# Gated linear attention: exponents formed on TensorE in PSUM, output weights as the loaded operand, decay applied to token rows, scores on 64-row halves, gate rows in three parts

## The chip, the cores and the metric

The kernel is one program on 1 core of one Trainium2 chip. The metric is the time of one execution on the device in microseconds, the median of several. The core has TensorE (PE; matmuls from SBUF into PSUM, each with a weight load shown as PEld), VectorE (DVE), ScalarE (ACT), GpSimd (POOL) and SyncE (SP, which here only starts DMAs). Each engine runs its own list of instructions in order; they meet at semaphores.

## The reference, cut to what matters

```python
# attention: q, k, v, o_gate (2, 8, 768, 40), i_gate, f_gate (2, 8, 768)
for t in range(S):
    m_new = np.maximum(f_gate[:, :, t] + m, i_gate[:, :, t])
    f_stab = np.exp(f_gate[:, :, t] + m - m_new)
    i_stab = np.exp(i_gate[:, :, t] - m_new)
    m = m_new
    C = f_stab[..., None, None] * C + i_stab[..., None, None] * einsum('bhd,bhe->bhde', vt, kt)
    n = f_stab[..., None] * n + i_stab[..., None] * kt
    h_tilde = einsum('bhde,bhe->bhd', C, qt)
    denom = np.maximum(np.abs(einsum('bhd,bhd->bh', n, qt)), 1.0)
    y[:, :, t] = sigmoid(o_gate[:, :, t]) * h_tilde / denom
# x = y with the heads side by side: (2, 768, 320)
h = np.maximum(x.T @ w_tok1, 0) @ w_tok2        # over tokens
u = x + h.T
u = u + np.maximum(u @ w_ch1, 0) @ w_ch2        # over channels, 1536 wide
gate = sigmoid(causal 5-tap convolution of u with conv_w)
out = (gate * (u @ w_val)) @ w_out
```

## The kernel before

**Attention.** The recurrence is done in chunks of 128 tokens: `NC` = 6 for each of the 2 batches; chunk `u` = 6 b + n. The 8 heads stand in two groups `g` of four: group 0 on rows 0 to 39, group 1 on rows 64 to 103. The gate rows, 16 heads by 768 tokens, are scanned by VectorE in two parts (`ROWS_PARTS`): `m_row` the running maximum, `G_row` the summed log decay since the chunk's start, `A_row` the log weight of each token, `W_row` the weight up to the chunk's end. `G_row` goes to DRAM and comes back broadcast to 128 rows (`G_all`). For each chunk then:

- VectorE forms the exponents of the 128x128 matrix of each head, `min(G_all + A_col, mask)`, eight instructions (L933); ScalarE takes the exponential (L697).
- TensorE forms scores from zero-padded 128-row `k_in` and `q_in` (L1209, in `s_ps`), VectorE multiplies them with the exponentials (L952, `prob`).
- The chunk's output is `hv_ps`, stored as 41 values (40 and the normaliser) by 128 tokens: the 41 columns of `v_in` (L1194) and of the state `apart` (L1190, against `qs`, the queries times `decay`, GpSimd L590) are loaded, `prob` or `qs` is streamed, group 1 writes PSUM rows 64 and up. ScalarE copies it (`ht`, L712), TensorE turns it (`turn_y`, L1230), VectorE normalises it (L972 to L982), GpSimd multiplies by the output gate (L602), and it is split into a rounded part and a rest (`y_hi`, `y_lo`).
- The state gets `wv` by keys (L1220, job `delta`) plus `kept`, the old state times the chunk's decay.

**The rest.** Token mixing (`token_hidden` L1246, `token_skip`, `token_mixed`), the channel products in steps of 128 of 1536 hidden channels (`channel_hidden` L1171, job `ch1`; `channel_out` L1309), then convolution, `val` and `out`. Each product is three fp32r products of hi and lo parts. Weights arrive in ten pieces and are split by ScalarE (hi) and VectorE or GpSimd (lo, `make_lo`).

**Order.** Everything is written out by hand. The first batch's attention runs first, with token products of finished chunks between; the second batch's seven attention steps stand behind every second channel step of the first quarter `q` = 0 (`ATT_AT`). Two PSUM banks `shared` are handed round in the order of the list of `shared_bank_jobs`: job number N waits at `begin` until job N-2 has been released with `took`.

## Time and profile before

| | us |
|---|---|
| median of 3 runs | 311.26 (309.58 to 311.6) |
| span of the profiled execution, first to last instruction | 308.2 |
| TensorE busy | 270.8 |
| VectorE busy | 210.7 |
| ScalarE busy | 121.9 |
| GpSimd busy | 89.4 |

The profiled execution is known by its span alone; what the device time has around it is the difference to the median, 3.1 us. A busy matmul time counts each matmul from its start to its modelled end, so overlapping ones look long; how far apart starts lie is the better price.

### The profile page before, as it was taken

Reading aid. Unit: us, or ns where it says so; the run is one execution under the profiler, and the core shown is the slowest. Engines: PE = TensorE matmul, PEld = TensorE weight load, DVE = VectorE, ACT = ScalarE, POOL = GpSimd, SP = SyncE. Lnnn points to the kernel's source line nnn. Section 1 sums busy time; section 2 is a strip of 40 time slices with the busy share of each in tenths; the row PEclk is TensorE's granted clock in tenths of the full one; section 3 lists DMA queues with packets and bytes.
Section 4 is the critical chain, followed back from the end, with each engine's and each line's share of the span. In section 5 each row is a group of like instructions: output and inputs, shape, how many; then the busy total and the mean of one; then the engine's idle time right before and its main releaser. Section 6 shows DMA issues by size and latency. Waiting matters only on the chain.

```text
span 308.2 us, 5374 instructions
## 1 busy us (share of the span) xinstructions
PE 270.8 (88%) x2024; PEld 258.5 (84%) x2024; DVE 210.7 (68%) x415; ACT 121.9 (40%) x224; POOL 89.4 (29%) x102
## 2 busy tenths in 40 slices
PE   0876765884999999999999999999999999999854
PEld 0765654783998999999899999999999999999754
DVE  7999999977778687576677740352774138763693
ACT  4344453432874453434434223323123333231623
POOL 4537445554046445334610400000004000040340
PEclk9999598796899999999999999999999999999999
DMA  7599833344547554242000001000000010000011
GB/s 223 158 309 310 241 128 83 100 170 144 169 128 217 141 155 117 66 136 65 2 0 0 3 0 66 0 0 2 0 2 1 32 34 0 2 0 1 23 43 64
DMA packets 26289, 25.70 MB, mean 83 GB/s; under 512 B 13976, under 2 KB 22008, under 8 KB 26264
## 3 DMA queue, kind: packets, MB, share of 16 engines
q1 hardware_dynamic: 21976, 18.72, 20.9%
q10 hardware_dynamic: 4288, 6.64, 6.5%
q8 instruction: 16, 0.26, 0.3%
q14 instruction: 9, 0.07, 0.1%
HBM read 23.34 MB, written 2.02 MB: 82 GB/s over the span
## 4 chain that ended last, share of the span: by engine, by line
PE 60%; DVE 17%; issue 7%; ACT 6%; DMA 4%; POOL 3%; SPq 1%; ACTq 0%; DVEq 0%; POOLq 0%
PE shared L1171 25%; PE h_ps L1309 18%; DVE prob L933 7%; PE s_ps L1209 3%; DVE gate L1037 2%; PE hv_ps L1190 2%; PE shared L1274 2%; PE s_ps L1246 2%; PE hv_ps L1194 2%; PE shared L1230 2%; DVE y_lo L942 1%; DMA G_all<-G_scratch 1%; PE shared L1259 1%; DMA stage<-val 1%; DMA stage<-wout 1%
## 5 line engine op out<-in xcount | busy, mean ns | idle before, releaser
L933 DVE SCALAR_TENSOR_TENSOR prob<-G_all,A_col,mask_sb 128x128 f32<-128x128 f32 x96 | 51.3, 602 | 0.2 <-DMA G_all<-G_scratch 0.2
L1101 DVE SCALAR_TENSOR_TENSOR h_lo<-shared,h_hi 128x384 fp32r<-128x384 f32 x48 | 26.5, 557 | 35.0 <-ACT h_hi L826 34.8
L1309 PE MATMUL h_ps<-ch_hi,h_hi 128*128 128x320 f32 x144 | 45.4, 315 | 0.0
L1309 PE MATMUL h_ps<-ch_hi,h_lo 128*128 128x320 f32 x144 | 44.5, 309 | 0.0
L826 ACT ACTIVATE h_hi<-shared 128x384 fp32r<-128x384 f32 x48 | 23.1, 488 | 53.8 <-PE shared L1171 50.8
L1309 PE MATMUL h_ps<-ch_lo,h_hi 128*128 128x320 f32 x144 | 44.3, 308 | 0.0
L697 ACT ACTIVATE prob<-prob 128x512 f32<-128x512 f32 x24 | 15.0, 631 | 48.5 <-DVE prob L933 48.4
L1171 PE MATMUL shared<-u_hi,ch_hi 128*128 128x384 f32 x96 | 32.9, 342 | 0.6 <-DVE yt L982 0.4
L1171 PE MATMUL shared<-u_lo,ch_hi 128*128 128x384 f32 x96 | 32.5, 339 | 0.0
L1171 PE MATMUL shared<-u_hi,ch_lo 128*128 128x384 f32 x96 | 32.5, 338 | 0.0
L1037 DVE SCALAR_TENSOR_TENSOR gate<-x,conv_sb,gate 128x384 f32<-128x384 f32 x44 | 29.0, 668 | 1.0
L1209 PE MATMUL s_ps<-q_in,k_in 128*128 128x128 f32 x192 | 27.2, 301 | 2.1 <-DMA q_in<-qT 2.1
L1209 PEld LDWEIGHTS s_ps<-q_in,k_in 128*128 128x128 f32 x192 | 25.3, 212 | 4.1 <-DMA q_in<-qT 2.2
L1309 PEld LDWEIGHTS h_ps<-ch_hi,h_hi 128*128 128x128 f32 x144 | 27.1, 188 | 0.4 <-DVE yt L982 0.2
L1309 PEld LDWEIGHTS h_ps<-ch_lo,h_hi 128*128 128x128 f32 x144 | 27.1, 188 | 0.0
L1309 PEld LDWEIGHTS h_ps<-ch_hi,h_lo 128*128 128x128 f32 x144 | 27.0, 188 | 0.0
L1194 PE MATMUL hv_ps<-prob,v_in 128*41 128x128 f32 x192 | 20.6, 309 | 2.3 <-DVE prob L952 2.3
L952 DVE TENSOR_TENSOR prob<-s_ps,prob 128x512 f32<-128x512 f32 x24 | 15.8, 686 | 7.4 <-PE s_ps L1209 7.1
L602 POOL TENSOR_TENSOR y<-yt,o_sig 128x320 f32<-128x320 f32 x11 | 11.4, 1033 | 31.3 <-DVE yt L982 31.3
L1171 PEld LDWEIGHTS shared<-u_hi,ch_hi 128*128 128x128 f32 x96 | 18.0, 188 | 1.5 <-DVE yt L982 0.7
L536 POOL TENSOR_TENSOR ch_lo<-stage,ch_hi 128x640 fp32r<-128x640 f32 (+1 forms) x8 | 13.2, 1661 | 20.7 <-ACT ch_hi L668 20.7
L1230 PE MATMUL shared<-ident_r,ht 105*128 105x105 f32 x48 | 7.4, 282 | 12.5 <-ACT ht L712 12.5
(189 smaller groups left out, 620.6 us busy)
## 6 DMA issues: line engine op xcount, KB each, us to landing
G_all<-G_scratch SPq DMA_DIRECT2D x11, 512.0 KB, 4.8
o_sig<-on ACTq DMA_DIRECT2D x2, 960.0 KB, 6.1
k_in<-kT SPq DMA_DIRECT2D x24, 80.0 KB
q_in<-qT SPq DMA_DIRECT2D x24, 80.0 KB
kn_in<-kn SPq DMA_DIRECT2D x12, 160.0 KB, 3.9
v_in<-vn SPq DMA_DIRECT2D x12, 160.0 KB, 4.6
stage<-ch ACTq DMA_DIRECT2D x3, 640.0 KB, 4.4
out<-o_sb SPq DMA_DIRECT2D x12, 160.0 KB, 1.8
```

The source lines that it names most:

```text
L536: eng.tensor_tensor(lo[:, half], raw[:, half], hi[:, half].bitcast(F32), ALU.subtract).then_inc(split[p], 1)
L697: act.activation(prob[w % 4][:], prob[w % 4][:], ACT.Exp).then_inc(exp_ready, 1)
L826: act.activation(h_hi[i % 3][:], ps_of(key)[:, 0:T], ACT.Relu).then_inc(hi_ready, 1)
L933: last = dve.scalar_tensor_tensor(out=prob[(2 * u + g) % 4][:, tile_cols(j)], in0=G_all[u % 2][:, tile_cols(h)], scalar=A_col[:, col:col + ...
L952: dve.tensor_tensor(prob[w % 4][:], s_ps[g][:], prob[w % 4][:], ALU.mult).then_inc(prob_ready, 1)
L1037: return dve.scalar_tensor_tensor(out=gate[:, d, :], in0=xt, scalar=w, in1=gate[:, d, :], op0=ALU.mult, op1=ALU.add)
L1101: took(dve.scalar_tensor_tensor(out=h_lo[i % 3][:], in0=ps_of(key)[:, 0:T], scalar=0.0, in1=h_hi[i % 3][:].bitcast(F32), op0=ALU.max, op1= ...
L1171: last = pe.matmul(out_ap, w, x, start=(n == 0), stop=(n == len(terms) - 1))
L1194: last = pe.matmul(hv_ps[64 * g:64 * g + D1, tile_cols(j)], v_in[v % 3][:, g * HG + j, :], prob[(2 * v + g) % 4][:, tile_cols(j)], start=( ...
L1209: last = pe.matmul(s_ps[g][:, tile_cols(j)], k_in[k_buffer(u)][:, g, tile_cols(j)], q_in[k][:, tile_cols(j)], start=True, stop=True)
L1230: last = pe.transpose(ps[:, j * P:j * P + 64 + D1], ht[:, tile_cols(j)], ident_f[0:64 + D1, 0:64 + D1])
L1309: last = pe.matmul(h2_ps[t][:, 0:DM], a[:, tile_cols(t)], w[:, f, :], start=(f == 0 and n == 0), stop=(f == FT - 1 and n == 2))
```

## The change

What it does, by part:

- **Exponents.** G_all, the DRAM round trip, A_col and the eight VectorE instructions go. TensorE adds the mask (identity loaded, mask streamed) and the two gate terms (`AB`, 66 rows, loaded; `MV`, 66 rows by 1024, streamed: head indicators and two flat rows with the rounded G and its rest, filled by two DMAs from `GH`). ScalarE reads the exponents from PSUM. The gate inputs are sent twice (48 rows), ScalarE and VectorE make the rounded parts.
- **Banks.** Exponents and scores of a chunk take four banks from a ring: three banks in the first batch, the two `s_ps` in the second.
- **Scores.** `k_in` loses its padding: each matmul uses 40 rows at row 0 or 64, groups in turn, two banks.
- **Output.** `prob` and `q_in` are loaded (128 columns), the 41 columns of `v_in` and of `state` are streamed; tokens are PSUM rows at once. Group 0 goes to `hv_ps`, group 1 to a shared bank (job `x`). `ht`, `turn_y`, `qs`, `apart`, `decay` go; VectorE multiplies the state part by the token's decay and adds it (`join`, four instructions), then `normalise` (seven).
- **Gate rows** are scanned in three parts (1, 1 and 4 chunks); the third stands on VectorE behind chunk 0's attention. A column of chunk decays `dl` comes from a small TensorE product.

```diff
@@ shared_bank_jobs
-        return ([("delta", u)] if n < NC - 1 else []) + ([("y", u - 1)] if n >= 1 else [])
+        return ([("x", u - 1)] if n >= 1 else []) + ([("delta", u)] if n < NC - 1 else [])
-ROWS_PARTS = ((0, 1), (1, NC))
+ROWS_PARTS = ((0, 1), (1, 2), (2, NC))
+        rings = [s_ps + h2_ps[2:3], s_ps]
+        def es_bank(u, i):
+            b, n = divmod(u, NC)
+            return rings[b][(4 * n + i) % len(rings[b])]
@@ SP
+            def G_chunk(u):
...
+                for r in range(2):
+                    sp.dma_start(MV[u % 2][64 + r:65 + r, :].bitcast(F32).rearrange("o (h l) -> o h l", l=L),
+                                 GH[32 * r + b * H:32 * r + (b + 1) * H, tile_cols(n)].bitcast(F32)
+                                 ).then_inc(G_flat[u % 2], 16)
@@ ScalarE
+            def rounded_rows(k):
...
+                act.wait_ge(G_ready, k + 1)
+                act.activation(GH[0:RP, cols], G_row[:, cols], ACT.Copy).then_inc(GH_hi, 1)
+                act.wait_ge(rows_ready, k + 1)
+                act.activation(AB[0][:, cols], A_row[:, cols], ACT.Copy,
+                               scale=cst[:, C_MASK:C_MASK + 1]).then_inc(AB_hi[0], 1)
+            def decays(k):
...
+                act.activation(ge[:, c0:c1], G_row[0:B * H]..., ACT.Exp).then_inc(ge_ready, 1)
             def exps(u):
...
+                    act.activation(prob[w % 4][:], es_bank(u, g)[:], ACT.Exp).then_inc(exp_ready, 1)
             def attention(b, n):
-                    act.activation(ht[:], hv_ps[0:64 + D1, :], ACT.Copy).then_inc(ht_ready, 1)
+                if n < NC:
+                    exps(u)
+                if u == 0:
+                    decays(1)
+                    columns(1)
+                    output_gate(0)
+                    rounded_rows(2)
+                    decays(2)
@@ VectorE
-                        last = dve.scalar_tensor_tensor(
-                            out=prob[(2 * u + g) % 4][:, tile_cols(j)], in0=G_all[u % 2][:, tile_cols(h)],
-                            scalar=A_col[:, col:col + 1], in1=mask_sb[:], op0=ALU.add, op1=ALU.min)
+            def join(v):
+                full(dve, ("x", v))
...
+                steps = [after(dve.tensor_tensor(tmp[g][:]..., x[:, 1],
+                                                 wd_col[:, 1, ...]..., ALU.mult))
+                         for g, x in enumerate(halves(v))]
+                for g, x in enumerate(halves(v)):
+                    dve.wait_ge(vector_step, steps[g])
+                    steps[g] = after(dve.tensor_tensor(x[:, 0], x[:, 0], tmp[g][:]..., ALU.add))
+            def normalise(v, steps):
...
+                took(last, ("x", v))
             def attention(b, n):
+                steps = join(u - 1) if n >= 1 else None
...
+                        dve.tensor_tensor(prob[w % 4][:], es_bank(u, 2 + g)[:], prob[w % 4][:],
+                                          ALU.mult).then_inc(prob_ready, 1)
+                if n >= 1:
+                    normalise(u - 1, steps)
...
+                if u == 0:
+                    gate_rows(2)
@@ TensorE
+            def exponents(u):
...
+                for g in range(2):
+                    ps = es_bank(u, g)
+                    pe.matmul(ps[:]..., ident_r[:], mask_r[:]..., start=True, stop=False)
+                    pe.matmul(ps[:], AB[b][:, tile_cols(n)], MV[u % 2][:, g * HG * L:(g + 1) * HG * L],
+                              start=False, stop=True).then_inc(e_ready, 1)
+            def scores(u):
...
+                for j in range(HG):
+                    for g in range(2):
+                        r = slice(64 * g, 64 * g + D)
+                        last = pe.matmul(es_bank(u, 2 + g)[:, tile_cols(j)], k_in[k][r, tile_cols(j)],
+                                         q_in[k][r, tile_cols(j)], start=True, stop=True)
+            def outputs(v):
+                banks = [hv_ps, begin(("x", v))]
+                if v >= 1:
+                    done(pe, ("x", v - 1))
+                if n >= 1:
...
+                            pe.matmul(banks[g][:, (HG + j) * D1:(HG + j + 1) * D1], q_in[k][r, tile_cols(j)],
+                                      state[(v - 1) % 2][r, j * D1:(j + 1) * D1], start=True, stop=True)
...
+                        last = pe.matmul(banks[g][:, j * D1:(j + 1) * D1], prob[(2 * v + g) % 4][:, tile_cols(j)],
+                                         v_in[v % 3][:, g * HG + j, :], start=True, stop=True)
             def attention(b, n):
+                exponents(u); outputs(u - 1); scores(u); state_step(u); token_hidden(0, n - 3)
```

(The last line puts the five calls of the new `attention` in a row; each has its bounds on n.)

TensorE, second batch, third attention step (behind channel step 4), before:

```order
L1190 MATMUL hv_ps<-qs_114,apart_118 41x128 x2
L1194 MATMUL hv_ps<-prob_110,v_in_104 41x128
L1194 MATMUL hv_ps<-prob_111,v_in_104 41x128
L1209 MATMUL s_ps<-q_in_97,k_in_99 128x128 x3
L1220 MATMUL shared<-wv,kn_in_101 64x41 x3
L1220 MATMUL shared<-wv,kn_in_101 40x41 x4
L1230 MATMUL shared<-ident_r,ht 128x105 x3
```

and now (L1245 and L1247 the exponents, L1280 the state part, L1286 the prob part, L1265 scores, L1299 the state update; after the channel output L1392 comes channel step 5, L1222):

```order
L1245 MATMUL s_ps<-mask_r,ident_r 128x512 [waits prob_ready]
L1247 MATMUL s_ps<-MV_108,AB_106 128x512
L1280 MATMUL hv_ps<-state_115,q_in_97 128x41
L1280 MATMUL shared<-state_115,q_in_97 128x41
L1286 MATMUL hv_ps<-v_in_103,prob_112 128x41 x3
L1286 MATMUL shared<-v_in_103,prob_113 128x41 x3
L1265 MATMUL s_ps<-q_in_96,k_in_98 128x128 x7
L1299 MATMUL shared<-wv,kn_in_100 64x41
L1299 MATMUL shared<-wv,kn_in_100 40x41
```

The transposes are gone, four wide matmuls stand ahead, and the output matmuls write 128 token rows instead of 41.

VectorE at the same step, before:

```order
L952 TENSOR_TENSOR prob_108<-s_ps,prob_108 128x512 [waits s_ready,exp_ready]
L952 TENSOR_TENSOR prob_109<-s_ps,prob_109 128x512 [waits s_ready,exp_ready]
L963 TENSOR_TENSOR state<-shared,kept 104x164 [waits kept_ready,apart_ready,shared_full]
L972 TENSOR_SCALAR den<-shared 128x8 [waits shared_full]
L942 TENSOR_TENSOR y_lo<-y_121,y_hi 128x384 [waits y_hi_ready]
L976 SCALAR_TENSOR_TENSOR den<-shared,den 128x8 [waits vector_step]
L979 RECIPROCAL rden<-den 128x8 [waits vector_step]
L982 TENSOR_TENSOR yt<-shared,rden 128x4x2x40 [waits y32_ready,vector_step]
```

and now:

```order
L985 TENSOR_TENSOR tmp_118<-hv_ps,wd_col 128x164 [waits shared_full]
L985 TENSOR_TENSOR tmp_119<-shared,wd_col 128x164
L991 TENSOR_TENSOR hv_ps<-hv_ps,tmp_118 128x164 [waits vector_step]
L991 TENSOR_TENSOR shared<-shared,tmp_119 128x164 [waits vector_step]
L1025 TENSOR_TENSOR prob_110<-s_ps,prob_110 128x512 [waits s_ready,exp_ready]
L1025 TENSOR_TENSOR prob_111<-s_ps,prob_111 128x512 [waits s_ready,exp_ready]
L1002 TENSOR_SCALAR den<-hv_ps 128x4 [waits vector_step]
L1005 SCALAR_TENSOR_TENSOR den<-hv_ps,den 128x4 [waits vector_step]
L1008 RECIPROCAL rden<-den 128x8 [waits vector_step]
L1012 TENSOR_TENSOR yt<-hv_ps,rden 128x160 [waits y32_ready,vector_step]
L1012 TENSOR_TENSOR yt<-shared,rden 128x160
```

`join` of the previous chunk stands ahead of the products, its normalisation behind them; the second L1012 releases the shared bank.

ScalarE between the first and the second chunk's exponentials, now (before, the sigmoid stood ahead of the first, and between them only `w_col` and `decay`):

```order
L722 ACTIVATE prob_111<-s_ps 128x512 [waits e_ready]
L698 ACTIVATE ge<-G_row 16x1
L706 ACTIVATE wd_col<-shared 128x2x16 [waits shared_full]
L683 ACT_TABLE_LOAD
L683 ACTIVATE o_sig<-o_sig 128x1920 [waits o_in]
L690 ACTIVATE GH<-G_row 48x512 [waits G_ready]
L692 ACTIVATE AB_105<-A_row,cst 66x512 [waits rows_ready]
L698 ACT_TABLE_LOAD
L698 ACTIVATE ge<-G_row 16x4
L722 ACTIVATE prob_112<-s_ps 128x512 [waits e_ready]
```

The exponentials of chunk 1 stand behind the third part's rounded rows and a table load.

## Rows read from the trace of the kernel before

**Rows 1.** The page's head: span, busy time of each engine.

```profile
span 308.2 us, 5374 instructions
...
PE 270.8 (88%) x2024; PEld 258.5 (84%) x2024; DVE 210.7 (68%) x415; ACT 121.9 (40%) x224; POOL 89.4 (29%) x102
```

**Rows 2.** Busy us (instructions) of PE, PEld, DVE, ACT, POOL by stretch; clock, DMA.

```profile
42.00:52.00 10.00, 5.98 (x74) 5.45 (x74) 9.86 (x20) 4.98 (x8) 5.45 (x6) 0.98 0.41 119
52.00:62.00 10.00, 8.10 (x60) 7.18 (x61) 9.58 (x20) 5.69 (x10) 4.34 (x4) 0.67 0.45 128
...
74.00:88.00 14.00, 14.00 (x75) 13.21 (x76) 9.98 (x22) 10.95 (x16) 0.00 (x0) 0.82 0.54 177
...
103.00:114.00 11.00, 11.00 (x107) 10.37 (x105) 7.92 (x19) 5.41 (x9) 5.17 (x6) 1.00 0.43 118
```

**Rows 3.** Timeline of VectorE, 31 to 43 us: start, us, instruction, count, idle before.

```profile
31.91 1.29 DVE L952 TENSOR_TENSOR prob<-s_ps,prob 128x512 f32<-128x512 f32 x2
33.12 0.32 DVE L963 TENSOR_TENSOR state<-shared,kept 104x164 f32<-104x164 f32 x1
...
34.48 0.20 DVE L979 RECIPROCAL rden<-den 128x8 f32<-128x8 f32 x1
34.72 0.49 DVE L982 TENSOR_TENSOR yt<-shared,rden 128x320 f32<-128x320 f32 x1
35.12 6.53 DVE L933 SCALAR_TENSOR_TENSOR prob<-G_all,A_col,mask_sb 128x128 f32<-128x128 f32 x8
...
42.09 1.29 DVE L952 TENSOR_TENSOR prob<-s_ps,prob 128x512 f32<-128x512 f32 x2
```

**Rows 4.** Timeline of GpSimd, 24 to 34 us.

```profile
28.75 1.79 POOL L536 TENSOR_TENSOR tok_lo<-stage,tok_hi 128x768 fp32r<-128x768 f32 x1
```

**Rows 5.** Timeline of TensorE's weight loads, 103.5 to 108.7 us.

```profile
103.70 0.16 PEld L1190 LDWEIGHTS hv_ps<-qs,apart 128*41 128x41 f32 x4 [0.25 <-issue]
...
105.58 1.86 PEld L1209 LDWEIGHTS s_ps<-q_in,k_in 128*128 128x128 f32 x16 [0.19 <-issue]
107.56 0.64 PEld L1220 LDWEIGHTS shared<-wv,kn_in 128*64 128x64 f32 x16
108.25 0.38 PEld L1230 LDWEIGHTS shared<-ident_r,ht 105*128 105x128 f32 x4
```

**Rows 6.** The chain that ended last, in order of time: start, us, what.

```profile
110.18 1.39 PE shared L1171 x8
111.57 1.31 PE h_ps L1309 x9
...
197.52 1.29 PE shared L1259 x12
```

**Rows 7.** Timeline of ScalarE, 80 to 92.5 us.

```profile
80.19 1.15 ACT L697 ACTIVATE prob<-prob 128x512 f32<-128x512 f32 x2
...
84.97 1.28 ACT L691 ACT_TABLE_LOAD   x1
```

**Rows 8.** Timeline of VectorE, 2 to 24 us.

```profile
5.55 1.53 DVE L891 TENSOR_TENSOR_SCAN m_row<-f_row,m_row,i_row 16x640 f32<-16x640 f32 x1
...
12.77 0.81 DVE L906 TENSOR_TENSOR W_row<-A_row,G_row 16x640 f32<-16x640 f32 x1
...
13.70 2.19 DVE L933 SCALAR_TENSOR_TENSOR prob<-G_all,A_col,mask_sb 128x128 f32<-128x128 f32 x8
15.81 1.47 DVE L952 TENSOR_TENSOR prob<-s_ps,prob 128x512 f32<-128x512 f32 x2
```

**Rows 9.** Timeline of TensorE's weight loads, 3 to 18 us.

```profile
8.24 3.49 PEld L1209 LDWEIGHTS s_ps<-q_in,k_in 128*128 128x128 f32 x16 [2.22 <-DMA q_in<-qT]
```

**Rows 10.** The page's DMA issues: count, KB each, us from issue to landing.

```profile
out<-o_sb SPq DMA_DIRECT2D x12, 160.0 KB, 1.8
```

**Rows 11.** Timeline of all engines, 68 to 74 us.

```profile
68.71 2.12 DVE L1004 TENSOR_TENSOR y<-yt,o_sig 128x320 f32<-128x320 f32 x1
...
73.77 0.63 PE L1246 MATMUL h_ps<-y_hi,tok_hi 128*128 128x320 f32 x1 [4.21 <-DVE y_lo L942]
```

More of the change, by code:

```diff
@@ L347, in with_both, with x_done @@
             return (NC - 2) * (u // NC) + min(u % NC, NC - 2)
-        def k_buffer(u):
-            return 1 if u < NC and u % 2 else 0
-        def k_users(u):
-            return [x for x in range(u + 1) if k_buffer(x) == k_buffer(u)]
+        def x_done(eng, u):
+            full(eng, ("x", u))
         def used_h(eng, n):
```

525 lines of the change are left out of this document (280 added, 245 removed).

## The prediction

> **What bounds the kernel now.** I read the page's head first [rows 1]: TensorE is busy 88% of 308.2 us, VectorE 68%. An average hides that the limits change, so next came the busy time by stretch [rows 2]. From 42 to 52 us (first batch's attention) VectorE is busy 9.86 of 10 us and TensorE 5.98. From 74 on TensorE has no idle time worth the name (14.00 of 14, 11.00 of 11) while VectorE sits near 70%. So there are two regimes: the first batch waits for VectorE, all later work for TensorE. A microsecond of VectorE saved pays only before 74 us; a microsecond of TensorE added costs one after it.
>
> The first batch, one chunk [rows 3]: from one product of scores and weights at 31.91 to the next at 42.09 is 10.2 us; 6.53 of them are the eight exponent additions of L933. At the very start the same eight take 2.19 [rows 8], so some 4.3 us are waits, and they fall where GpSimd works: the last of its tensor operations of the chunk before still runs from 28.75 to 30.5 [rows 4]. The products that read PSUM are not held up (1.29 for two, both times).
>
> The second batch, one chunk on TensorE [rows 5]: `hv` 103.70 to 105.58 = 1.88, scores 1.98, state update 0.69, transposes 0.38: 4.9 us, between the channel products of 1.39 and 1.31 per step [rows 6]; two steps and a chunk make 10.3.
>
> **The change on TensorE, one full chunk.** *Exponents*: four new matmuls over 512 columns. Eight of 384 columns take 1.39 [rows 6], 0.174 each, so 512 take 0.23 and four 0.92. *Prob part of the output*: the 128-wide weights become the loaded operand. Each fp32 product is two load/matmul pairs, so 16 pairs. Twelve pairs with a 128-wide load and little to stream take 1.29 [rows 6], 0.11 each: 1.76 us. Before, with 41-wide loads and two column halves side by side, the whole `hv` group is 32 pairs in 1.88, 0.059 each [rows 5]. *State part*: 16 pairs, now on the two 64-row halves. *Scores*: 16 pairs, also on halves, against 1.98 before. No row of before shows row halves. Bounds: 0.043 a pair as the state update has (0.69 for 16, with loads of 64 and 40), or 0.11 as if one after the other (1.76 for 16). I take 0.059 (0.94), because the column halves are the nearest row with two tiles at work; the lower end would save 0.5 us a chunk. *State update* stays 0.69, transposes go (-0.38). Changes of tile shape show 0.2 us of idle each in [rows 5] (0.25 and 0.19); there are one or two more, 0.3 us. Sum: 0.92 + 0.94 + 1.76 + 0.94 + 0.69 + 0.3 = 5.6 us, +0.7; with serial halves 7.3, +2.4.
>
> One rule speaks against this edit. The Trainium skill, TensorEngine Tiling (Array Packing), Performance Considerations, advises for a narrow streamed operand (free size up to 64) to swap it into the stationary place and tile by columns. That is the kernel before; the change undoes it for the 41-wide values, and the trace agrees with the rule ([rows 5] against [rows 6]): 0.059 against 0.11. On the halves, the Trainium skill, TensorE: Matmul & The Clock Gate, Part 3, reports 3.07 times the speed for four row tiles at 512 columns; by it the halves overlap and the chunk's sum is 5.6, without it 7.3. No row here shows that.
>
> Over the second batch's seven steps (first has no output, second no state part, sixth no update, seventh only the output) the TensorE work comes to -0.1 + 0.7 + 3 x 0.7 + 0.6 + 0.6 = +3.9 us (serial halves: +13).
>
> **A new wait.** The output of chunk u-1 now sits in a shared bank, and the next channel step's bank is the same one (jobs: ch1 i, x, delta, ch1 i+1). It is freed by the last instruction of `normalise`, which VectorE runs after `join` and after both products of chunk u. From the end of the outputs: signal 0.2; join, four PSUM operations of 128x164, nearest L963 at 0.32: 1.25; two products 1.3; normalise: five small ones, nearest the reciprocal at 0.20, partly overlapping, two halves of `yt` at about 0.3 (L982 is 0.49 for both at once), with gaps 1.55 [rows 3]. Sum 4.3. TensorE meanwhile has scores, update and one channel_out: 0.1 + 0.94 + 0.69 + 0.1 + 1.31 = 3.1. It stands 1.2 to 1.3 us, with channel step, channel_out and all of the later work queued behind. Before, that bank belonged to the state update, freed right after the product. Times: 1.0 (second step, no join) + 3 x 1.3 + 0.5 (sixth, a channel step more as cover) = 5.4 us. In the first step TensorE also forms exponents and then needs both exponentials before the scores, since only two banks serve both; ScalarE has to take h_hi (about 0.5), a table load (1.28) and two exponentials (1.15 for two) [rows 7], 3.3 us with signals, TensorE has 0.9 to fill: +2.4. Second batch: 3.9 + 5.4 + 2.4 = +11.7 us. That VectorE loses its L933 work there is worth nothing; it is hidden already.
>
> **The first batch.** L933 goes, but a ring appears: outputs(v) -> join(v) -> products(v+1) -> normalise(v) -> outputs(v+1), because `hv_ps` is single and freed by normalise. 2.7 to 2.95 + 0.2 + 1.25 + 1.3 + 1.55 + 0.2 = 7.5 us a chunk against 10.2. TensorE fills most of the gap (scores, update, token products, exponents, 3.5 us), so I expect 2.4 GHz. VectorE's GpSimd waits shrink to y_lo, all else reads PSUM.
>
> The start changes twice [rows 8]. G no longer goes through DRAM: the first gate part ends at 5.6, its rounding and scheduling take about 0.7, a DMA 1.8 [rows 10] and a second issue 0.4, so exponents start near 8.6 instead of 13.7; 0.9 for a cold group, 0.2, 0.65, scores 1.8 (16 pairs took 3.49 at 1.2 GHz [rows 9], halved by the halves), 0.2, 1.3: first products done near 13.8 instead of 17.3. But then, from 14.3, VectorE does the third part of the gate rows: 640 columns took 5.55 to 13.58, 8.0 us, so 512 take 6.5: W_row at about 21. Behind it ScalarE rounds A_row 0.6, loads a table 1.28, only then exps(1) at 23.1 to 23.8, then scores(1), cold again, 1.8, and products done at 27.2 against 23.7. On TensorE scores end at 25.6, then cold state update 1.2 (twice 0.69 at most), column transposes 1.3 (ten at 0.11, partly cold), exponents(2) 1.3, outputs(1) 2.95: end at 32.4. Four rings on, outputs(5) end at 62.4. The tail: join and normalise 3.2, make_lo 1.75, y_lo 0.55, y32 0.5 to 3.9 (L1004 alone 2.12, beside GpSimd's weight halves), rounding and y_lo 1.2, 8.4 us with 0.7 for y32: token product of the last chunk at 70.8 instead of 73.77 [rows 11]: -3. If the halves are serial: +1.8 twice at the start, +0.9, and 1.6 a ring: 81.8, +8. The stretch from there to the second batch is TensorE's in both (14.00 of 14), nothing changes. After 157 no instruction changes.
>
> **Sum.** 308.2 [rows 1] - 3 + 11.7 = 316.9 us of span. The median is 3.1 above the profiled span (311.26 against 308.2), so 320.
>
> **Rivals.** (a) *Serial row halves*: +13 of work, stalls 5.8 (more cover), first batch +8: 308.2 + 26.8 + 3.1 = 338. For it: separate loads of 128 columns each seem to cost 0.11 in every row. Against: column halves do overlap. (b) *Faster*: the VectorE chain between outputs and the freed bank takes at most 3.1 us, not 4.3 (PSUM to PSUM additions of 164 overlapping as two products do, normalise under 1.0). Then the bank wait vanishes (-5.4), the ring is 6.3 (-5 more in the first batch), leaving 320 - 10.4 = 309.6; with the start 3 us better as well (gate rows not held up by GpSimd) 306.6. It decides at 3.1 us. Against: the small operations have rows. (c) *Cold ring*: TensorE stays at 1.2 GHz in the first batch, as 52 to 62 partly does (granted 0.67 [rows 2]); outputs 5.4 for 2.7, scores +0.9: +3.5 a ring, four rings: 333. Against: gaps of 1 us, not 4. (d) Half of (b): 312.
>
> **How the numbers follow.** Forecast 320 with 0.5, (a) 0.2, (b) 0.12, (c) 0.08, (d) 0.1. The range leaves out (b)'s lower part and the top end: 309 to 339. A measurement here tells about 1% from no change (308.1 to 314.4): faster 0.12, same 0.13, slower 0.75.
>
> **What would show it.** In the profile after: L1265 16 pairs in about 1.0 us (a: 1.9); L1280 likewise; L1286 16 in 1.8; TensorE idle of 1.3 us before L1222 on L1012 once a chunk between 85 and 145; first token product of the last chunk near 71; rings of 7.5 us between L1025 pairs; VectorE's busy time down by some 45 us. I am wrong if TensorE has no idle time after 85, if the ring is 6 us, or if the first products of chunk 2 come before 33.

## The result, and the profile after

The changed kernel takes 349.84 us (median of 4 runs, 345.91 to 350.95), the kernel before on the same chip 311.18 (309.58 to 311.6): 12.9% slower, ratio 1.1291, 95% interval 1.1216 to 1.1366. The page's head after, which answers to [rows 1]:

```profile
span 344.1 us, 5324 instructions
...
PE 307.7 (89%) x2032; PEld 291.0 (85%) x2032; DVE 174.2 (51%) x387; ACT 108.3 (31%) x205; POOL 73.1 (21%) x91
```

VectorE lost 36.5 us of work and the span gained 35.9, with 8 matmuls more than before (2032 for 2024). Two marks divide it: the first channel step of the second batch begins at 110.07 (86.35 before), and the last channel output of `q` = 0 ends at 185.48 (148.48 before). So the first batch lost 23.7 us, the second batch's attention 13.3 (75.4 against 62.1), and what follows gave 1.1 back. These are marks of one profiled execution each; that of the changed kernel is its fastest (345.91).

**The first batch.** Busy time by stretch, with the columns of [rows 2]; the column behind GpSimd's is the granted clock:

```profile
42.00:52.00 10.00, 10.00 (x68) 8.70 (x67) 5.86 (x15) 1.76 (x4) 4.10 (x5) 1.00 0.48 147
```

VectorE no longer bounds this stretch (5.86 for 9.86), TensorE does (10.00 for 5.98). VectorE's timeline, as in [rows 3]:

```profile
45.02 0.69 DVE L1025 TENSOR_TENSOR prob<-s_ps,prob 128x512 f32<-128x512 f32 x1 [1.05 <-PE h_ps L1265]
...
47.23 0.32 DVE L1012 TENSOR_TENSOR yt<-shared,rden 128x160 f32<-128x160 f32 x1
...
55.48 0.69 DVE L1025 TENSOR_TENSOR prob<-h_ps,prob 128x512 f32<-128x512 f32 x1 [1.05 <-PE s_ps L1265]
```

From products to products it is 10.46 us; the eight additions of L933 are gone and the chunk is no shorter. A chunk now goes round a ring: its outputs wait for the normalisation of the chunk before, and that stands behind products which wait for TensorE's scores. TensorE's weight loads show why (a row's busy time runs from its first start to its last end):

```profile
46.44 0.33 PEld L1245 LDWEIGHTS s_ps<-mask_r,ident_r 128*128 128x128 f32 x1
46.87 0.33 PEld L1247 LDWEIGHTS s_ps<-MV,AB 66*128 66x128 f32 x1
47.85 0.28 PEld L1280 LDWEIGHTS hv_ps<-state,q_in 40*128 40x128 f32 x1 [0.65 <-DVE yt L1012]
...
49.71 1.78 PEld L1286 LDWEIGHTS hv_ps<-v_in,prob 128*128 128x128 f32 x8
...
69.27 1.78 PEld L1265 LDWEIGHTS s_ps<-q_in,k_in 40*128 40x128 f32 x16
```

Two matmuls of 512 columns start 0.43 apart, which is the 1.2 GHz level (0.23 apart at 144 us). Eight pairs of the prob part take 1.78 us, 16 score pairs 1.78. The same groups in the second batch:

```profile
146.56 0.97 PEld L1286 LDWEIGHTS hv_ps<-v_in,prob 128*128 128x128 f32 x8
147.44 0.97 PEld L1286 LDWEIGHTS shared<-v_in,prob 128*128 128x128 f32 x8
148.47 0.97 PEld L1265 LDWEIGHTS s_ps<-q_in,k_in 40*128 40x128 f32 x16
149.56 0.54 PEld L1299 LDWEIGHTS shared<-wv,kn_in 128*64 128x64 f32 x16
```

So this turn of the ring is outputs 5.4, scores 2.1, products 1.2, normalisation 1.4 and signals, all of TensorE's share at the lower level, and TensorE's one gap over 0.3 us in it is 0.65. The four turns from the end of chunk 1's outputs to the end of chunk 5's take 10.5, 16.0, 9.2 and 10.1 us; the second holds the wait for `tok_lo` shown below, and in the third the clock was up for a short while (75.5 to 78.4).

**The start**, which answers to [rows 8]. VectorE's third part of the gate rows, TensorE's columns, and ScalarE:

```profile
17.64 1.28 DVE L921 TENSOR_TENSOR_SCAN m_row<-f_row,m_row,i_row 48x512 f32<-48x512 f32 x1
...
23.30 1.11 DVE L936 TENSOR_TENSOR W_row<-A_row,G_row 48x512 f32<-48x512 f32 x1
```

```profile
21.42 0.85 PE L1440 MATMUL shared<-gm,cst 16*104 16x4 f32 x4 [4.24 <-POOL gm L566]
```

```profile
22.52 1.28 ACT L683 ACT_TABLE_LOAD   x1
23.81 1.80 ACT L683 ACTIVATE o_sig<-o_sig 128x1920 f32<-128x1920 f32 x1
25.52 0.61 ACT L690 ACTIVATE GH<-G_row 48x512 fp32r<-48x512 f32 x1
...
28.17 0.57 ACT L722 ACTIVATE prob<-s_ps 128x512 f32<-128x512 f32 x1
```

GpSimd's little product `gm` stands behind its subtraction for the third part, TensorE's columns wait for it, ScalarE's sigmoid for them. The exponentials of chunk 1 begin at 28.17, its products at 31.10 (22.4 before), its outputs end at 42.83. Once more in the first batch TensorE stands still, for GpSimd's second half of `tok_lo`:

```profile
60.23 0.64 PE L1329 MATMUL h_ps<-y_hi,tok_hi 128*128 128x320 f32 x1 [3.87 <-POOL tok_lo L535]
```

The last chunk's outputs end at 88.5. TensorE then waits for the `y_lo` of the chunk before (93.33), makes that chunk's token product and twelve matmuls of `token_skip`, and only then the last chunk's token product, 23.7 us later than before (73.77):

```profile
97.44 0.33 PEld L1329 LDWEIGHTS h_ps<-y_hi,tok_hi 128*128 128x128 f32 x1
```

**The second batch**, which answers to [rows 5, 6]. The channel step after an attention step, and the step in which the clock fell:

```profile
152.32 0.19 PEld L1222 LDWEIGHTS shared<-u_hi,ch_hi 128*128 128x128 f32 x1 [0.86 <-DVE yt L1012]
```

```profile
158.59 0.97 PEld L1286 LDWEIGHTS hv_ps<-v_in,prob 128*128 128x128 f32 x8
...
160.59 1.78 PEld L1265 LDWEIGHTS s_ps<-q_in,k_in 40*128 40x128 f32 x16
162.60 0.93 PEld L1299 LDWEIGHTS shared<-wv,kn_in 128*64 128x64 f32 x16 [0.22 <-issue]
163.61 0.29 PEld L1392 LDWEIGHTS h_ps<-ch_hi,h_hi 128*128 128x128 f32 x1
```

The awaited wait for the shared bank is there, 0.86 us, but in two steps only. In two others the clock went from 2.4 to 1.2 GHz in the middle of TensorE's own work (at 136 and at 160), right behind the prob part, with no wait before it. In the first step it fell as well, at 116, there behind the wait of 2.54 us for the exponentials.

### The profile page after: what moved, and what is told of

It reads as the page before. It is cut to its first block, busy times and chain, and to the rows that moved or that the text cites. A ratio compares the mean times of both kernels' runs of the same rounds, so it can differ in the third digit from the quotient of the medians.

```text
span 344.1 us, 5324 instructions
## 1 busy us (share of the span) xinstructions
PE 307.7 (89%) x2032; PEld 291.0 (85%) x2032; DVE 174.2 (51%) x387; ACT 108.3 (31%) x205; POOL 73.1 (21%) x91
## 4 chain that ended last, share of the span: by engine, by line
PE 80%; DVE 5%; ACT 4%; issue 3%; POOL 1%; ACTq 0%; DVEq 0%; POOLq 0%
PE shared L1222 26%; PE h_ps L1392 18%; PE s_ps L1265 5%; PE hv_ps L1286 4%; PE shared L1286 4%; PE hv_ps L1280 4%; PE h_ps L1329 3%; PE shared L1342 2%; PE shared L1357 2%; PE shared L1299 2%; PE s_ps L1329 2%; PE s_ps L1245 1%; PE s_ps L1247 1%; PE s_ps L1512 1%; PE shared L1404 1%
## 5 line engine op out<-in xcount | busy, mean ns | idle before, releaser
L1392 PE MATMUL h_ps<-ch_hi,h_hi 128*128 128x320 f32 x144 | 46.4, 322 | 0.0
L1392 PE MATMUL h_ps<-ch_hi,h_lo 128*128 128x320 f32 x144 | 45.2, 314 | 0.0
L1392 PE MATMUL h_ps<-ch_lo,h_hi 128*128 128x320 f32 x144 | 45.1, 313 | 0.0
L1222 PE MATMUL shared<-u_hi,ch_hi 128*128 128x384 f32 x96 | 33.6, 350 | 1.2 <-DVE yt L1012 1.2
L1222 PE MATMUL shared<-u_lo,ch_hi 128*128 128x384 f32 x96 | 33.1, 345 | 0.0
L1222 PE MATMUL shared<-u_hi,ch_lo 128*128 128x384 f32 x96 | 33.0, 344 | 0.0
L1392 PEld LDWEIGHTS h_ps<-ch_hi,h_hi 128*128 128x128 f32 x144 | 27.7, 193 | 0.6 <-DVE h_lo L1152 0.2
L1392 PEld LDWEIGHTS h_ps<-ch_lo,h_hi 128*128 128x128 f32 x144 | 27.8, 193 | 0.0
L1392 PEld LDWEIGHTS h_ps<-ch_hi,h_lo 128*128 128x128 f32 x144 | 27.7, 193 | 0.0
L1265 PE MATMUL s_ps<-q_in,k_in 40*128 40x128 f32 x160 | 20.7, 366 | 3.5 <-ACT prob L722 3.5
L985 DVE TENSOR_TENSOR tmp<-hv_ps,wd_col 128x164 f32<-128x164 f32 x10 | 3.3, 328 | 37.5 <-PE shared L1286 37.5
L1265 PEld LDWEIGHTS s_ps<-q_in,k_in 40*128 40x128 f32 x160 | 17.6, 260 | 4.5 <-issue 4.0
L1222 PEld LDWEIGHTS shared<-u_hi,ch_hi 128*128 128x128 f32 x96 | 18.6, 193 | 2.2 <-DVE yt L1012 1.7
L1025 DVE TENSOR_TENSOR prob<-s_ps,prob 128x512 f32<-128x512 f32 x20 | 13.1, 686 | 14.3 <-PE s_ps L1265 11.9
L1222 PEld LDWEIGHTS shared<-u_lo,ch_hi 128*128 128x128 f32 x96 | 18.5, 192 | 0.0
L1222 PEld LDWEIGHTS shared<-u_hi,ch_lo 128*128 128x128 f32 x96 | 18.5, 192 | 0.0
L535 POOL TENSOR_TENSOR ch_lo<-stage,ch_hi 128x640 fp32r<-128x640 f32 (+1 forms) x8 | 12.9, 1628 | 21.3 <-ACT ch_hi L678 21.3
L1280 PEld LDWEIGHTS hv_ps<-state,q_in 40*128 40x128 f32 x80 | 12.9, 242 | 5.3 <-issue 4.4
L1286 PE MATMUL shared<-v_in,prob 128*128 128x41 f32 x96 | 17.1, 339 | 0.0
```

The costliest lines, as they stand in the source:

```text
L535: eng.tensor_tensor(lo[:, half], raw[:, half], hi[:, half].bitcast(F32), ALU.subtract).then_inc(split[p], 1)
L1025: dve.tensor_tensor(prob[w % 4][:], es_bank(u, 2 + g)[:], prob[w % 4][:], ALU.mult).then_inc(prob_ready, 1)
L1222: last = pe.matmul(out_ap, w, x, start=(n == 0), stop=(n == len(terms) - 1))
L1265: last = pe.matmul(es_bank(u, 2 + g)[:, tile_cols(j)], k_in[k][r, tile_cols(j)], q_in[k][r, tile_cols(j)], start=True, stop=True)
L1280: pe.matmul(banks[g][:, (HG + j) * D1:(HG + j + 1) * D1], q_in[k][r, tile_cols(j)], state[(v - 1) % 2][r, j * D1:(j + 1) * D1], start=True ...
L1286: last = pe.matmul(banks[g][:, j * D1:(j + 1) * D1], prob[(2 * v + g) % 4][:, tile_cols(j)], v_in[v % 3][:, g * HG + j, :], start=True, st ...
```

## The experiments

Times are medians; "first batch" ends with the first channel step (110.07 in the changed kernel), "second" is the length of its attention up to the last channel output (75.4), and "falls" counts how often the granted clock went down in it behind the first attention step. These three are from the one profiled execution of each kernel. The kernel before took 310.0 to 311.3 us beside each of these runs.

| kernel | us | first batch | second | falls |
|---|---|---|---|---|
| before | 311.2 | 86.35 | 62.1 | 0 |
| changed | 349.8 | 110.07 | 75.4 | 2 |
| e1 prob streamed | 339.2 | 103.58 | 74.2 | 0 |
| e2 prob part twice | 369.7 | 113.22 | 93.1 | 4 |
| e3 other start | 349.4 | 108.69 | 80.1 | 4 |
| e4 tok_lo first | 343.7 | 105.66 | 78.5 | 3 |
| e5 before + halves | 311.4 | 87.00 | 62.6 | 1 |
| e6 two parts | 342.7 | 104.40 | 80.0 | 4 |
| e7 = e6 + e4 | 334.4 | 94.57 | 77.9 | 2 |
| e8 = e7 + e1 | 325.8 | 92.35 | 74.2 | 0 |
| e9 output back | 321.7 | 94.26 | 69.1 | 0 |
| e10 = e7 + wide matmuls | 334.5 | 87.23 | 80.1 | 4 |
| e11 = e9 grouped | 304.9 | 87.36 | 65.2 | 0 |
| e12 = e11 + wide matmuls | 307.1 | 80.31 | 65.2 | 0 |
| e13 = e7 + wide once | 338.4 | 99.01 | 75.4 | 2 |
| e14 = e11 + wide once | 305.0 | 87.72 | 65.2 | 0 |

The column of falls is the plainest finding. Eight kernels keep the changed prob part (128 columns loaded, 41 streamed) in the second batch: 25 falls, each within the output's matmuls or at most 1.2 us behind them. Six others of these kernels load 41 columns and stream 128 there (e1, e8, e9, e11, e12, e14): no fall. Granted clock, last column but two, of the changed kernel and of e1 behind the first step:

```profile
119.50:185.50 66.00, 64.80 (x530) 60.44 (x529) 29.73 (x93) 16.82 (x33) 17.69 (x22) 0.92 0.21 55
```

```profile
115.00:178.00 63.00, 60.63 (x527) 54.86 (x527) 29.88 (x94) 16.34 (x32) 17.65 (x22) 1.00 0.22 58
```

**e1, the prob part streamed.**

```diff
-  pe.matmul(banks[g][:, j * D1:(j + 1) * D1], prob[...][:, tile_cols(j)], v_in[v % 3][:, g * HG + j, :], ...)
+  pe.matmul(banks[g][0:D1, 328:456], v_in[v % 3][:, g * HG + j, :], prob[...][:, tile_cols(j)], ...)   # v >= 2
```

> From the third chunk on the prob part of the output is issued with the operands in the other places: the 41 columns of v_in are loaded, the 128 of prob are streamed (into columns of the bank that nothing reads, so the output's values leave that part out). Number of matmuls, waits and order stay; a pair should cost the same 0.11 us at 2.4 GHz and 0.21 at 1.2. Theory A (the shape with 128 columns loaded for 41 streamed is what holds TensorE at 1.2 GHz): the rings of the first batch fall from 10.4 us to 7.0 to 7.5 us, the two falls of the clock in the second batch (scores of 1.8 us at 160, channel outputs of 2.06 and 2.37 us) vanish, and the time is 335 to 339. Rival B (the waits in the ring, some 1 to 4 us each, are what keep the clock low, whatever is issued between them): rings stay at 10.4, time 348 to 351.

339.16 us (337.8 to 342.95), 10.7 less, just above theory A's 335 to 339. Rows of TensorE's loads in a ring and in a step of the second batch:

```profile
64.93 0.81 PEld L1290 LDWEIGHTS hv_ps<-prob,v_in 128*41 128x41 f32 x8
...
66.80 0.97 PEld L1265 LDWEIGHTS s_ps<-q_in,k_in 40*128 40x128 f32 x16 [0.19 <-issue]
...
146.80 0.19 PEld L1222 LDWEIGHTS shared<-u_hi,ch_hi 128*128 128x128 f32 x1 [0.85 <-DVE yt L1012]
```

The ring is 6.76 us (63.91 to 70.67), and no step of the second batch behind the first falls. In the first batch the clock still fell, each time around a wait of TensorE (5.3 us for `tok_lo` ahead of 60.31, 1.7 at 77.5, 2.8 ahead of 87.5), and once more behind the wait for the exponentials in the second batch's first step. So waits go with falls too; Rival B, by which they alone decide and the rings stay at 10.4, is out, since TensorE waits more for `tok_lo` here, not less. The first two rings, however, are hardly shorter (13.93 and 9.82 us between products, for 13.92 and 10.46): only from 53.7 on is TensorE at 2.4 GHz. In the second batch the four steps now each show the wait of 0.85 to 0.88, so only 1.2 us are gained there against the changed kernel's profiled execution: what the low clock had cost had also been the cover of that wait. Against e3, e4, e6, e7, e10 and e13, whose second batch is that of the changed kernel, it is 1.2 to 5.9.

**e2, the prob part twice** (each of its matmuls of the second batch issued two times).

> In the second batch alone each matmul of the prob part is issued twice, 16 pairs more in six steps. TensorE hardly waits there. Theory A (this shape takes the clock down): the clock falls in every one of these steps, so that beside the 6 x 1.8 = 10.8 us of added work the scores, the state update and the next channel output run at 1.2 GHz (+1.0, +0.4, +0.8 us and part of the added work itself): 20 to 28 us more than the changed kernel, 370 to 378. Rival B (the clock falls for waits): the added work covers the two waits for the bank (0.87 us each), the clock stays, 9 to 11 us more, 359 to 361.

369.7 us (366.55 to 372.42): 19.9 more for 10.8 of work. The clock fell in four of the six steps (two of the changed kernel's), as here:

```profile
174.24 1.87 PEld L1286 LDWEIGHTS shared<-v_in,prob 128*128 128x128 f32 x16
176.15 1.79 PEld L1265 LDWEIGHTS s_ps<-q_in,k_in 40*128 40x128 f32 x16
178.16 0.93 PEld L1299 LDWEIGHTS shared<-wv,kn_in 128*64 128x64 f32 x16 [0.23 <-issue]
```

Both sides of theory A hold in the second batch: without the shape no falls, with twice as much of it four. (Four falls also stand in e3, e6 and e10 with the shape once, so that the number varies between executions.)

**e3, the start in another order** (PE: `exponents(1)` ahead of `columns(1)`; ACT: `exps(1)` ahead of `columns(1)`, `output_gate(0)` behind `decays(2)`; DVE: the third part's rests behind the products of chunk 1).

> The start in another order: TensorE forms the exponents of chunk 1 ahead of the columns of the second gate part, ScalarE takes their exponentials right behind those of chunk 0 and the sigmoid of the output gate after the third part's rounding, VectorE makes the rounded rests of the third part only after the products of chunk 1. Theory C (the order at the start costs 5 us of what was lost): the products of chunk 1 come at 25 to 26 instead of 31.1, everything after moves up with them, time 343 to 345. Rival: what comes next (the bank that columns of part 3 waits for, GpSimd's second half of tok_lo at 58.4, which the whole of TensorE waited for) is late by itself and takes the gain back: 348 to 350.

349.38 us (346.78 to 349.63), nothing gained. The scores of chunk 1 came 3.4 us earlier (25.43), the exponents of chunk 2, which need the third part, only 1.9, and the first token product, behind `tok_lo`, 1.4 (58.87). The second batch of its profiled run was 4.7 us longer. The rival was right.

**e4, tok_lo first.**

```diff
+                if b == 0 and (b, n) in LO_POOL_AT:
+                    make_lo(pool, *LO_POOL_AT[b, n])
                 if 1 <= n < NC - 1:
                     pool.wait_ge(dl_ready, ...)      # kept, weigh
```

> GpSimd makes each half of tok_lo ahead of the chunk's kept and weigh instead of behind them, in the first batch. Theory D (the 3.9 us in which TensorE waits for the second half of tok_lo at 56.3 to 60.2 are lost once and for all): the second half is done before 52, TensorE goes on at 56.4, time 345 to 346. Rival: kept and weigh come 1.8 us later now and hold the state update, so that each ring gains that and the time is 349 to 352; or the wait is only replaced by one for VectorE's y_lo, beside GpSimd's work, 348 to 350.

343.74 us (three runs at 343 to 345 and one at 336.88), 6.1 less, where I had expected 4 to 5; the profiled first batch is 4.4 shorter. Theory D holds: the token product follows the state update at once, at 55.86 instead of 60.23, and `kept`, now behind `tok_lo`, held nothing up.

**e5, the kernel before with the scores on halves alone** (`k_in[r, g]` and `q_in[r]` for `r` of 40 rows, both banks in turn).

> The kernel before with one part of the change alone: the scores on the two 64-row halves, both banks in turn (40 rows of the padded k_in and of q_in each, 16 matmuls as before). If halves overlap and nothing else comes with them, the scores of a chunk take 0.97 us instead of 1.86 in the second batch, six times, with one change of tile shape that was there already: -5.3 us, 305 to 307. Rival: the clock falls through them (40 of 128 rows at work) and the time is 311 to 316, as it would be if the halves alone were what took the clock down in the changed kernel.

311.43 us against 310.89 (12 and 17 runs), ratio 0.9974 (0.9915 to 1.0034): no difference. The scores did halve, and the rows behind them show where the 0.9 us went:

```profile
115.92 0.97 PEld L1209 LDWEIGHTS s_ps<-q_in,k_in 40*128 40x128 f32 x16 [0.19 <-issue]
119.33 0.64 PEld L1221 LDWEIGHTS shared<-wv,kn_in 128*64 128x64 f32 x16 [2.44 <-DVE h_lo L1101]
```

```profile
110.35 7.29 DVE L933 SCALAR_TENSOR_TENSOR prob<-G_all,A_col,mask_sb 128x128 f32<-128x128 f32 x8
```

Two steps were 9.65 us instead of 10.5, in another TensorE waited for VectorE, whose eight additions took 7.29 beside GpSimd's work (3.85 at the same place before). The recorded clock also fell once, behind that wait and not behind the halves. So the halves by themselves cost TensorE nothing, and in the second batch VectorE seems to have been hidden by little more than the 0.9 us saved; that this took all of the gain is argued from one execution of each kernel.

**e6, gate rows in two parts; e7, that and tok_lo first; e8, that and prob streamed.**

```diff
-ROWS_PARTS = ((0, 1), (1, 2), (2, NC))
+ROWS_PARTS = ((0, 1), (1, NC))
@@ ScalarE
-            rounded_rows(1)
+            output_gate(0)          # ahead of exps(0); rounded_rows(1) behind it
```

> The changed kernel with the gate rows in two parts (1 and 5 chunks, both at the start) instead of three, and the sigmoid of the output gate ahead of the first exponentials, as both stood before. Theory C (the third part on VectorE, with the roundings, the sigmoid, the table load and the columns behind it, is what made the start late): the products of chunk 0 come at 18 to 20 (17.2 now), those of chunk 1 at 25 to 27 instead of 31.1, the outputs of chunk 1 at 29 to 31 instead of 37.4; 6 to 8 us gained, 342 to 344. Rival: GpSimd's second half of tok_lo (it waits for the state product and a load of v_in) takes it back as it did with the other order of the start, 347 to 350.

> The same, and tok_lo ahead of kept and weigh on GpSimd. Theory C and D together (both losses are lost once and stand behind each other): -6 to -8 for the start and -4 to -6 for tok_lo, 335 to 339. Rival (the ring of outputs, scores, products and normalisation at 1.2 GHz is all that counts after the start): 342 to 345.

> The same, and the prob part streamed from the third chunk on (the output's values leave it out, as in e1). If the three causes (clock, start, tok_lo) are all there is to the first batch's loss they add up: -10 for the clock, so 324 to 329, with the second batch's first channel step at 88 to 92 (86.4 before, 110.1 changed). Rival: a fourth cause, a transfer (k, q, v of the next chunks, which are sent only when outputs are done) or a weight piece, is next; then the first channel step comes at 95 or later and the time is 331 or more.

342.7 (340.08 to 344.8), 334.41 (332.04 to 337.93) and 325.8 us (325.63 to 327.12). In e6 the products of chunk 0 come at 19.27, 3.3 later than with three parts, those of chunk 1 at 28.50 instead of 31.10, and the outputs of chunk 1 at 31.29 instead of 37.40: theory C, though the products came later than I expected. e6 undoes two things, the third part and the place of the sigmoid; e3, which moved the sigmoid and kept the third part, gained nothing. The three causes add up: -10.7 (e1), -6.1 (e4) and -7.1 (e6) alone, -24.0 together. Where the clock was up in e8's first batch its rings took 6.76 and 6.78 us (53.24, 60.00, 66.78). The two before them took 10.42 and 10.45 between products, as in the changed kernel.

**e9, the output's operands put back; e11, the same grouped.** From e7, with everything else of the change kept (exponents on TensorE, scores on halves):

```diff
+  pe.matmul(ps[0:ROWS, :], sel[g], MV[u % 2][:, g * 512:(g + 1) * 512], start=(g == 0), stop=(g == 1))   # job "dec"
+  act.activation(decay[:], ps_of(("dec", u))[0:ROWS, :], ACT.Exp)
+  pool.tensor_tensor(q_in[u % 2][0:ROWS], q_in[u % 2][0:ROWS], decay[:], ALU.mult)     # after the scores
+  pe.matmul(hv_ps[64 * g:64 * g + D1, tile_cols(j)], state[(v - 1) % 2][r, ...], q_in[k][r, tile_cols(j)], ...)
+  pe.matmul(hv_ps[64 * g:64 * g + D1, tile_cols(j)], v_in[v % 3][:, g * HG + j, :], prob[...][:, tile_cols(j)], ...)
```

`ht`, `turn_y` and the one normalisation of before follow. e9 issues state and prob part in turns for each `j`, e11 all of the state part first.

> The part of the change that the runs point at is undone, the others kept: in e7's kernel (gate rows in two parts, tok_lo early) the output is again 41 values by 128 tokens, v_in and the state (40 rows at 0 or 64) loaded, prob and the decayed queries streamed, copied by ScalarE, turned by four transposes and normalised behind the state update. The decay of the queries comes from two more matmuls of 512 columns (the two flat rows of MV against ones), an exponential and one GpSimd product. The exponents of the second batch's first chunk are formed while TensorE waits for the last y_lo. Theory A: no shape with 128 loaded for 41 streamed is left, so TensorE stays at 2.4 GHz wherever it doesn't wait; nor does normalise hold a bank that the next channel step needs. A chunk of the first batch 6.5 to 7.5 us, first channel step of the second batch at 79 to 84 (86.4 before), a step pair of the second batch 10.6 to 10.9 (10.5 before, 12.0 with the changed output and the clock kept), time 303 to 309, better than before. Rival (the 66-row and 40-row matmuls take the clock down as well, or GpSimd with the decayed queries is next): rings of 8 to 10 us, time 312 to 325.

> e9's kernel with the output's matmuls in another order: all 16 of the state part (40 rows), then all 16 of the prob part (128 rows), instead of in turns head by head. In e9 each change between the two stood as 0.19 us of idle TensorE at 2.4 GHz and 0.36 at 1.2, seven changes fewer a chunk. Theory A with this price: a step pair of the second batch 10.5 instead of 11.85, five or six times, and 2.5 us a ring in the first batch while the clock is low there: 305 to 312, about the kernel before. If something else made e9's rings long, 318 to 322.

e9: 321.66 us (312.02 to 323.99), 13 to 19 more than I expected. No fall of the clock in the second batch and no wait for a bank, but a pair of steps took 11.85 us: between the 40-row and the 128-row matmuls TensorE stood 0.19 us each time, eight times a chunk, 0.36 at 1.2 GHz. A change, second batch of e9:

```profile
124.98 0.16 PEld L1317 LDWEIGHTS hv_ps<-prob,v_in 128*41 128x41 f32 x4 [0.19 <-issue]
125.34 0.15 PEld L1313 LDWEIGHTS hv_ps<-q_in,state 40*41 40x41 f32 x4 [0.19 <-issue]
```

e11, second batch:

```profile
105.90 0.81 PEld L1313 LDWEIGHTS hv_ps<-q_in,state 40*41 40x41 f32 x16 [0.39 <-issue]
106.90 0.81 PEld L1318 LDWEIGHTS hv_ps<-prob,v_in 128*41 128x41 f32 x16 [0.19 <-issue]
107.90 0.97 PEld L1285 LDWEIGHTS s_ps<-q_in,k_in 40*128 40x128 f32 x16 [0.19 <-issue]
```

Two parts of the output in 1.8 us where the changed kernel needs 2.9, and the pair of steps in 11.07 (102.84 to 113.91), 0.78 less than in e9 and not the 1.35 that I expected: a change costs about 0.11 us, less than the idle time that stands beside it. The Trainium skill, TensorEngine Tiling (Array Packing), Key Properties, says that a change of the tiling mode drains TensorE; these gaps agree. e11 takes 304.88 us (300.34 to 313.39) against 309.96, ratio 0.979 (0.9705 to 0.9875): faster than both kernels, by 1.3 to 3.0% of the kernel before. Its profiled execution was its slowest run, with its first rings at 1.2 GHz although nothing in it loads 128 columns for 41 streamed:

```profile
37.93 0.69 DVE L1049 TENSOR_TENSOR prob<-s_ps,prob 128x512 f32<-128x512 f32 x1 [6.40 <-PE h_ps L1285]
...
48.17 0.69 DVE L1049 TENSOR_TENSOR prob<-h_ps,prob 128x512 f32<-128x512 f32 x1 [6.96 <-PE s_ps L1285]
```

**e10, wide matmuls added to e7; e12, to e11; e13 and e14, once.**

```diff
-  pe.matmul(ps[:]..., ident_r[:], mask_r[:]..., start=True, stop=False)
+  for last_one in [False, False, True]:       # first batch from chunk 1 on (e10, e12); chunk 1 alone (e13, e14)
+      pe.matmul(ps[:]..., ident_r[:], mask_r[:]..., start=True, stop=not last_one)
```

> e7's kernel with work added in the first batch alone: from the second chunk on the mask's matmul (identity loaded, 512 columns streamed) is issued three times instead of once for each group, the first two being overwritten; 20 wide matmuls more, 0.21 us each at 2.4 GHz, 0.43 at 1.2. If more streamed columns bring the clock back in the ring (theory A from the other side), the rings of 10.4 us fall to 8 to 9 in spite of the added 0.85 us, and the time is 328 to 333. If the clock stays low whatever is put between the output's matmuls, each ring gains 1.0 to 1.7 us: 340 to 343.

> The same with the mask's matmul issued three times for each group from the second chunk of the first batch on, as in e10, where it took the rings of the first batch from 10.4 to 6.9 us. If more streamed columns ahead of the output bring the clock up here as well, the first batch's rings are 6.5 to 7.2 us throughout, the second batch's first channel step comes at 80 to 84, and the time is 298 to 304, 2 to 4% better than the kernel before. If the clock was up without them, they cost their 0.85 us a chunk where nothing waits: up to 4 us more than e11.

> e10's kernel with the four added mask products ahead of chunk 1's exponents alone. If the output's shape takes the clock down again and again (as in three of seven steps of the second batch, where TensorE had been at 2.4 GHz), the first batch begins at 2.4 GHz and falls back within a chunk or two: 332 to 341, near e7. If a cold start is all, the rings stay at 6.8 us as in e10, without its 0.85 us a chunk: 322 to 326.

> e11's kernel (the output of before, exponents on TensorE, two parts) with the same four products ahead of chunk 1's exponents alone. Here no shape of 128 loaded for 41 streamed is left, so by theory A what the four products bring stays: 302 to 305, the best of all, and steady. If the clock falls back here too, 304 to 313 with e11's spread.

e10's runs lie apart: 323.0, 327.7, 341.3 and 341.5. The profiled one (327.68) has the clock up from chunk 1's outputs (25.4) to 49, and 20 matmuls more made its first batch 7.3 us shorter than e7's (one execution each):

```profile
31.73 0.97 PEld L1280 LDWEIGHTS hv_ps<-v_in,prob 128*128 128x128 f32 x8
...
35.32 0.53 PEld L1239 LDWEIGHTS s_ps<-mask_r,ident_r 128*128 128x128 f32 x3
...
38.60 0.97 PEld L1280 LDWEIGHTS hv_ps<-v_in,prob 128*128 128x128 f32 x8
```

6.87 us from ring to ring. e13 (338.36, 335.11 to 340.57) got nothing from four matmuls once: the outputs right behind them still took 3.75, and the first rings were at 1.2 GHz and not, as I had expected, at 2.4. Later its clock did rise, and fell again behind the prob part, with no wait between:

```profile
55.81 0.97 PEld L1280 LDWEIGHTS hv_ps<-v_in,prob 128*128 128x128 f32 x8
56.70 1.42 PEld L1280 LDWEIGHTS shared<-v_in,prob 128*128 128x128 f32 x8
58.20 1.78 PEld L1259 LDWEIGHTS s_ps<-q_in,k_in 40*128 40x128 f32 x16
```

So the clock falls behind this shape time and again, also here in the first batch. e12 is the steadiest (305.95 to 310.25 in 12 runs, 307.07; ratio 0.9922, 0.9884 to 0.996) and its first batch is 6 us shorter than before's, its first two rings taking 6.56 us, but it missed my 298 to 304 and is no better than e11. e14: 305.04 (303.6 to 315.08), ratio 0.9843 (0.9788 to 0.9898), with the first rings of the profiled run at 1.2 GHz again (10.23 and 10.16 us).

## Why the prediction was wrong

Slower was right; 320 and the top of the range, 339, were too low. The span was 344.1 for 316.9, and the missing 27.2 us lie as follows:

| stretch | predicted | measured | off by |
|---|---|---|---|
| to the end of chunk 1's outputs | 32.4 | 42.8 | +10.4 |
| four rings, to the end of chunk 5's outputs | 30.0 | 45.7 | +15.7 |
| tail, to the last chunk's token product | 8.4 | 8.9 | +0.5 |
| from there to the second batch, against before | 0 | +0.1 | +0.1 |
| second batch, against before | +11.7 | +13.3 | +1.6 |
| the rest, against before | 0 | -1.1 | -1.1 |

By its own steps:

- **TensorE's sizes held.** Exponents of a chunk about 0.9 us; prob part 1.86 for 1.76; state part and scores 0.97 each for 0.94; a pair of steps +0.6 of work for +0.7. The row halves overlap, so rival (a) is out. The advice of the Trainium skill, TensorEngine Tiling (Array Packing), Performance Considerations, to swap a narrow streamed operand into the stationary place and tile by columns, holds here: the output's two parts take 1.81 us in e11 and 2.87 in the changed kernel.
- **The second batch held in its sum, in part by luck:** +13.3 for +11.7. First step: 2.54 of waiting for 2.4. The bank: 0.86 for 1.2 to 1.3, since two matmuls and a normalisation are a little quicker than added up, and in two steps where the clock had fallen not at all. The falls, which I had not foreseen, filled the place of the waits that did not come. With the clock kept (e1, e8) it is 74.2, +12.1, of which the four bank waits are 3.4.
- **The step that failed is "TensorE fills most of the gap (scores, update, token products, exponents, 3.5 us), so I expect 2.4 GHz".** It filled the gap and ran at 1.2 GHz: the ring 10.45 us instead of 7.5, the largest part of the 15.7 us above. That was rival (c), +3.5 a ring (measured +2.95), to which I gave 0.08, "against: gaps of 1 us, not 4". I judged the clock by the idle time alone. Whether TensorE was at 2.4 GHz in the rings is shown to be what counts: with the clock up and four wide matmuls more they take 6.83 and 6.87 us (e10). Why it was not is shown in part. The falls after a rise follow the shape (e1, -10.7 us by the shape alone, e13, and the second batches). The low level of the first two rings does not: they take 10.2 to 10.5 us in e8, e11 and e14 as well. At 2.4 GHz the ring is 6.8, for 7.5: products 1.2 for 1.3, normalisation with its signal about 1.4 for 1.75, and from outputs to products, where the scores cover `join`, 1.3 for 1.45.
- **The start was mis-sized.** The first exponents began at 11.8, not 8.6: TensorE waited for the flat rows of `MV`, whose DMAs could be issued only at 9.04, since ScalarE had rounded G at 8.41, behind the identity and the mask. So the first products, done at 17.3 as before, gained nothing of the 3.5 us expected. W_row of the third part ended at 24.41, not 21; the exponentials of chunk 1 began at 28.17, not 23.1, since the sigmoid with its table load, held by GpSimd's `gm`, stood in front. Then the step that I left out: the columns of the third part stand on TensorE ahead of the exponents of chunk 2, and their bank is freed by the normalisation of chunk 0 (33.6). Outputs of chunk 1 end at 42.83 for 32.4. e6 took 6.1 us of that back (outputs of chunk 1 at 31.29) by undoing the third part, which buys 3.3 us for the products of chunk 0 alone, and by putting the sigmoid first again.
- **Not in the prediction at all:** the wait of 3.87 us for `tok_lo`. On GpSimd `kept` now waits for the state product of its own chunk, and `tok_lo` stands behind it; I priced GpSimd's operations and not the order of its waits. e4: -6.1 us.
- **The tail** was 8.9 us (88.5 to 97.44) for 8.4, but the terms given for it add up to 7.4. TensorE, not VectorE, ended it: the `y_lo` of the last chunk was done at 95.26, and the matmuls of `token_skip`, at 1.2 GHz, stood in front of its product.

The three together (e8, 325.8) leave 14.6 us over the kernel before; in the profiled executions it is 17.1, of which 12.1 in the second batch as forecast, 6.0 in the first, and 1.0 back behind them. What stays open: why the clock is low in the first rings of every profiled kernel that has the exponents on TensorE and no added wide matmuls in each ring, with the shape and without it (e9, e11, e14). In e12 and in e10's profiled run, which have them, it is up there; which of the other matmuls or waits keep it down is not shown. In the changed kernel it rises at 75, in e7 with the same shape at 52, so that the waits taken out there may have a part in it. And that e11's quicker runs have the clock up early was not seen in a profile.

## What to carry to other kernels

Cost a matmul group at both levels of TensorE's clock, and after changing an operand's shape read the level from the trace: a TensorE that is busy throughout can still sit at the lower one (10.00 of 10 us here). Work taken off an engine pays only until the next thing in the ring, and a wait can be hidden by another loss, so undo parts one by one and together before naming a cause. When a part of a scan or a list is moved, follow every small instruction that stands behind it on each queue (`gm`, the columns, the sigmoid, `tok_lo`), since these cost more here than the matmuls.
